# Decays counted from a chunk's first token, receptance and state split into fp16 parts, increments added before the decay

## The reference

```python
for t in range(S):
    cur = einsum('bhd,bhe->bhde', u[None] * kt, vt)
    y[:, :, t] = einsum('bhd,bhde->bhe', rt, state + cur)
    state = wt[:, :, :, None] * state + einsum('bhd,bhe->bhde', kt, vt)
```

## Time and profile before

| what | us |
|---|---|
| median of 3 runs | 421.21 |
| lowest and highest | 420.39, 424.6 |
| span of the profiled execution | 418.7 |
| busy PE, DVE, POOL, ACT | 402.8, 338.7, 187.7, 162.3 |

### The profile page before, as it was taken

How to read it: one execution, slowest core, us unless ns; L and a number is a source line. 1 busy time by engine, 2 the same in 40 slices (tenths; PEclk the granted TensorE clock), 3 DMA queues, 4 the chain that set the end, 5 groups by cost and what they waited for, 6 DMA issues and landing times.

```text
span 418.7 us, 9789 instructions
## 1 busy us (share of the span) xinstructions
PE 402.8 (96%) x3913; PEld 220.6 (53%) x3913; DVE 338.7 (81%) x561; ACT 162.3 (39%) x299; POOL 187.7 (45%) x178
## 2 busy tenths in 40 slices
PE   8999999999999999999999999999999999999981
PEld 3885555555555555555555555455453444544430
DVE  7998799998998888989989998989975787662152
ACT  3586255533343244144433433351333234321141
POOL 4445988865465655445743556464450012010000
PEclk9999999999999999999999999999999999999996
DMA  8997321468043123314430331331006189869929
GB/s 250 358 398 274 123 83 43 124 237 291 21 124 123 55 71 125 97 29 124 125 112 13 122 102 36 112 122 59 0 4 261 43 347 419 257 254 415 407 106 358
DMA packets 16541, 69.35 MB, mean 166 GB/s; under 512 B 2160, under 2 KB 3184, under 8 KB 14832
## 3 DMA queue, kind: packets, MB, share of 16 engines
q1 hardware_dynamic: 16496, 68.73, 46.9%
HBM read 64.00 MB, written 4.72 MB: 164 GB/s over the span
## 4 chain that ended last, share of the span: by engine, by line
issue 36%; PE 26%; POOL 22%; DVE 7%; DMA 5%; ACT 1%; POOLq 0%; SPq 0%; DVEq 0%
POOL att L1552 5%; DMA att<-rkT_dram 4%; POOL att L1514 4%; PE hid L578 4%; POOL att L1516 4%; PE hid L580 4%; PE hid L579 4%; POOL att L1537 3%; POOL att L1570 3%; POOL w_split L1528 3%; PE hid L846 3%; PE hid L827 1%; PE sc_ps L827 1%; DVE gated L1009 1%; PE l_ps L626 1%
## 5 line engine op out<-in xcount | busy, mean ns | idle before, releaser
L1361 ACT ACTIVATE relu<-hid,three 128x512 f32<-128x512 f32 x95 | 65.1, 686 | 136.5 <-PE hid L580 136.2
L578 PE MATMUL hid<-x_split,w_split 128*128 128x512 f16 x285 | 108.3, 380 | 0.5 <-DVE gated L1009 0.4
L580 PE MATMUL hid<-x_split,w_split 128*128 128x512 f16 x285 | 108.0, 379 | 0.0
L579 PE MATMUL hid<-x_split,w_split 128*128 128x512 f16 x285 | 108.0, 379 | 0.0
L1009 DVE SCALAR_TENSOR_TENSOR gated<-relu,hid 128x512 f32<-128x512 f32 x95 | 64.3, 677 | 22.0 <-ACT relu L1361 21.3
L1030 DVE STREAM_TRANSPOSE ring<-gated 128x512 f32<-128x512 f32 x96 | 68.3, 711 | 3.3
L1543 POOL TENSOR_TENSOR att<-att 128x1024 f16<-128x1024 f32 x20 | 40.9, 2046 | 49.1 <-ACT att L1296 49.1
L1561 POOL TENSOR_TENSOR att<-att 112x512 f32<-112x512 f32 x19 | 23.2, 1222 | 55.8 <-DVE att L928 55.8
L578 PEld LDWEIGHTS hid<-x_split,w_split 128*128 128x128 f16 x285 | 27.7, 97 | 37.3 <-DVE gated L1009 6.8
L580 PEld LDWEIGHTS hid<-x_split,w_split 128*128 128x128 f16 x285 | 27.8, 98 | 33.7
L579 PEld LDWEIGHTS hid<-x_split,w_split 128*128 128x128 f16 x285 | 27.9, 98 | 24.9 <-issue 0.3
(11 more groups left out here) (276 smaller groups left out, 759.6 us busy)
## 6 DMA issues: line engine op xcount, KB each, us to landing
att<-nat_dram SPq DMA_DIRECT2D x20, 576.0 KB, 4.2
att<-rkT_dram SPq DMA_DIRECT2D x22, 448.0 KB, 5.6
att<-wT_dram SPq DMA_DIRECT2D x22, 226.2 KB, 4.8
att<-w_dram SPq DMA_DIRECT2D x3, 1536.0 KB, 9.7
out_dram<-w_split SPq DMA_DIRECT2D x11, 384.0 KB, 3.9
att<-w_dram SPq DMA_DIRECT2D x5, 768.0 KB, 10.7
stage<-w_in_dram SPq DMA_DIRECT2D x2, 1536.0 KB, 13.2
ring<-w_outT_dram SPq DMA_DIRECT2D x1, 3072.0 KB, 15.2
```

The source lines that it names most:

```text
L578: pe.matmul(hid[s % 2][:], high, x_high, start=(q == 0), stop=False)
L579: pe.matmul(hid[s % 2][:], high, x_low, start=False, stop=False)
L580: last = pe.matmul(hid[s % 2][:], low, x_high, start=False, stop=(q == KT - 1))
L1361: nc.scalar.activation(relu_tile(s), hid[s % 2][:], ACT.Relu, bias=three[:], scale=GATE / H_SCALE)\
```

## The change

The forward scan now comes first (phase 1) and starts at `R_SCALE` from `mark`; the reciprocal of its chunk totals starts the backward scan, which comes second (phase 3). So `decay_receptance(n + 1)` moves to phase 2 of POOL and `decay_keys(n + 1)` to phase 3. The receptance product has one buffer; ACT makes its fp16 high part in phase 0 (`high_receptance`), POOL its low part in phase 0 after `diag_products` (`low_receptance`, 112 x 512). ACT saves the chunk's decay in phase 2 (`save_decay`, 112 x 4). `decay_state(n - 1)` now works on a state to which the increment was already added, still in phase 3 of POOL, and after it comes `low_state(n - 2)` (112 x 384), whose high part ACT makes in phase 2 (`high_state`, 112 x 384). `attend` replaces each fp32 product by three fp16 products of the same 96 columns.

```diff
             def attend(n):
-                pe.wait_ge(decayed, n - B + 1)
+                pe.wait_ge(state_lo_done, n - B + 1)
+                pe.wait_ge(r_lo_done, n - B + 1)
...
-                    pe.matmul(both, r_dec[n % 2][0:PD, p * P:(p + 1) * P], state[b][0:PD, p, :],
-                              start=True, stop=False, skip_group_check=True)
+                    tokens = slice(p * P, (p + 1) * P)
+                    pe.matmul(both, r_hi[0:PD, tokens], state_hi[b][0:PD, p, :], start=True, stop=False,
+                              skip_group_check=True)
+                    pe.matmul(both, r_hi[0:PD, tokens], state_lo[b][0:PD, p, :], start=False, stop=False,
+                              skip_group_check=True)
+                    pe.matmul(both, r_lo[0:PD, tokens], state_hi[b][0:PD, p, :], start=False, stop=False,
+                              skip_group_check=True)
...
+            def scan_prefix(n):
+                dve.wait_ge(w_rows_in[n % B], 16 * (n // B + 1))
+                if n:
+                    dve.wait_ge(r_dec_done, n)
+                    dve.wait_ge(decay_saved, n)
+                nc.vector.tensor_tensor_scan(prefix[0:PD, :], w_rows_of(n)[0:PD, :], mark[0:PD, :], 1.0,
+                                             ALU.mult, ALU.add).then_inc(prefix_done, 1)
...
+            def scan_suffix(n):
+                dve.wait_ge(restart_done, n + 1)
+                if n:
+                    dve.wait_ge(k_dec_done, n)
+                nc.vector.tensor_tensor_scan(suffix[0:PD, ::-1], w_rows_of(n)[0:PD, ::-1], restart[0:PD, ::-1], 1.0,
+                                             ALU.mult, ALU.add).then_inc(suffix_done, 1)
...
+            def save_decay(n):
+                act.wait_ge(prefix_done, n + 1)
+                if n >= B:
+                    act.wait_ge(decayed, n - B + 1)
+                nc.scalar.activation(chunk_decay[n % B][0:PD].rearrange("p (i o) -> p i o", o=1),
+                                     pairs(prefix[0:PD, 0:TOTAL_COLS], P + 1)[:, :, P:P + 1], ACT.Copy,
+                                     scale=1.0 / R_SCALE).then_inc(decay_saved, 1)
+            def high_receptance(n):
+                act.wait_ge(r_dec_done, n + 1)
+                if n > B:
+                    act.wait_ge(y_ready, n)
+                nc.scalar.activation(r_hi[0:PD], r_dec[0:PD], ACT.Copy).then_inc(r_hi_done, 1)
+            def high_state(n):
+                act.wait_ge(decayed, n + 1)
+                if n >= B:
+                    act.wait_ge(y_ready, n + 1)
+                nc.scalar.activation(state_hi[n % B][0:PD], state[n % B][0:PD], ACT.Copy).then_inc(state_hi_done, 1)
...
+            def low_receptance(n):
+                pool.wait_ge(r_hi_done, n - B + 1)
+                nc.gpsimd.tensor_tensor(r_lo[0:PD], r_dec[0:PD], r_hi[0:PD], ALU.subtract).then_inc(r_lo_done, 1)
...
+            def low_state(n):
+                pool.wait_ge(state_hi_done, n + 1)
+                nc.gpsimd.tensor_tensor(state_lo[n % B][0:PD], state[n % B][0:PD], state_hi[n % B][0:PD], ALU.subtract)\
+                    .then_inc(state_lo_done, 1)
...
             for n in range(B):
-                decay_keys(n + 1)
+                decay_receptance(n + 1)
...
-            decay_state(B)
-            decay_keys(B + 1)
+                if n >= 2:
+                    decay_state(n - 2)
+            low_state(0)
+            decay_state(2)
+            low_receptance(B)
+            low_state(1)
+            decay_receptance(B + 1)
             diag_products(B)
             low_scores(B)
-            decay_receptance(B + 1)
+            decay_keys(B + 1)
             diag_values(B)
...
                 if phase == 0 and is_unit(n):
                     diag_products(n)
+                    low_receptance(n)
...
                 if phase == 2:
                     if n + 1 < UNITS:
-                        decay_keys(n + 1)
+                        decay_receptance(n + 1)
                 if phase == 3:
                     if n + 1 < UNITS and n > B:
-                        decay_receptance(n + 1)
+                        decay_keys(n + 1)
                     if is_unit(n) and n > B:
                         diag_values(n)
-                    if n + 1 < UNITS:
-                        decay_state(n + 1)
+                    if n - 1 < LAST_INC:
+                        decay_state(n - 1)
+                    if n - 2 < LAST_INC:
+                        low_state(n - 2)
```

More of the change, by code:

```diff
@@ L71, in build_program @@
         suffix, prefix, restart, mark = (carve(SCAN) for _ in range(4))
-        r_dec = [carve(PB * P) for _ in range(2)]
+        r_dec = carve(PB * P)
+        r_hi, r_lo = (carve(PB * P // 2).bitcast(F16) for _ in range(2))
         k_dec = [carve(PB * P) for _ in range(2)]
@@ L116, in build_program @@
         last_max = stats[:, 7:8]
+        chunk_decay = [stats[:, i:i + PB] for i in (32, 36, 64, 68)]
+        state_hi, state_lo = ([pairs(spare[:, first + b * PB * D:first + (b + 1) * PB * D].bitcast(F16), 2 * D) for b in range(B)]
+                              for first in (2 * PB, 2 * PB + B * PB * D))
         w_early = {2: gated[:, 0:SCAN], 3: relu[:, 0:SCAN]}
@@ L251, in build_program @@
         r_dec_done = sem("r_dec_done")
+        decay_saved = sem("decay_saved")
+        r_hi_done = sem("r_hi_done")
+        r_lo_done = sem("r_lo_done")
         decayed = sem("decayed")
+        state_hi_done = sem("state_hi_done")
+        state_lo_done = sem("state_lo_done")
         state_added = sem("state_added")
@@ L479, in score @@
                         rows = slice(ALIGN * j, ALIGN * j + D)
-                        last = pe.matmul(sc_bank[j][:, cols], k_dec[n % 2][rows, cols], r_dec[n % 2][rows, cols],
+                        last = pe.matmul(sc_bank[j][:, cols], k_dec[n % 2][rows, cols], r_dec[rows, cols],
                                          start=True, stop=True)
@@ L904, in receptance_of @@
         def receptance_of(n):
-            return pairs(r_dec[n % 2][0:PD, :], P), pairs(rk_rows_of(n)[0:PD, 0:PB * P], P), \
+            return pairs(r_dec[0:PD, :], P), pairs(rk_rows_of(n)[0:PD, 0:PB * P], P), \
                 pairs(prefix[0:PD, 0:TOTAL_COLS], P + 1)[:, :, 0:P]
@@ L1124, in _ @@
             dve.wait_ge(dve_consts, 2)
[L1125 to L1126 removed]
+            nc.vector.memset(pairs(mark[:, 0:TOTAL_COLS], P + 1)[:, :, 0:1], R_SCALE).then_inc(dve_consts, 1)
             dve.wait_ge(dve_consts, 3)
             dve.wait_ge(pool_consts, 2)
+            scan_prefix(0)
+            restart_suffix(0)
             scan_suffix(0)
[L1130 to L1131 removed]
             decay_keys(0)
@@ L1411, in _ @@
             make_fold()
+            save_decay(0)
             copy_keys(0)
@@ L1415, in _ @@
             for n in range(B):
+                save_decay(n + 1)
                 if 1 <= n and n + 1 < B:
@@ L1430, in _ @@
                 if n == 2:
+                    high_state(0)
                     high_w(2)
                     scale_w(2)
+            save_decay(B + 1)
+            high_receptance(B)
+            high_state(1)
             high_v(B)
             high_scores(B)
+            high_state(2)
             for s in range(END):
@@ L1453, in _ @@
                         copy_keys(n)
+                    if n + 1 < UNITS:
+                        save_decay(n + 1)
+                    if n - 2 < LAST_INC:
+                        high_state(n - 2)
                 if s < STEPS - 1:
```

72 lines of the change are left out of this document (31 added, 41 removed).

## The result

| | before | after |
|---|---|---|
| median, us | 420.8 (4 runs beside those of after) | 437.48 (437.04 to 440.11) |
| span of the profiled execution | 418.7 | 436.1 |

The ratio is 1.040, 95% interval 1.036 to 1.044. I had forecast 427.7 and a range of 413 to 432: the direction was right, the size outside the range. Each time is about 1.7 us above the span of the same execution.

A forecast was written before the change was run, and what follows sets the result against it. It took PE and an equally long DVE, POOL, ACT loop to bind together: 2.8 + 3.9 + 3.9 - 2.9 - 1.2 = +6.5 us on 418.7, plus 2.5 from span to median, gave 427.7 us; range 413 to 432.

The forecast's parts named there:

- Two loops of one length: Per unit, PE's work and a DVE, POOL, ACT loop without PE bind together; most of PE's 11.6 us saving is lost.
- Pace of PE: In attention, three fp16 products take 0.13 us, saving 0.145 us a pair, 11.6 us for 20 units of 4 pairs.
- Conversions on POOL: The added `low_state` and `low_receptance` on POOL take 0.83 and 1.05 us, 1.88 us a unit.
- Rival 1: In plain units `low_state` takes over 0.93 us, so DVE's scan comes first and loses nothing: 422.4 us, chance 0.24.
- Seven plain units, +3.9: Seven units after the first group each get 0.55 us longer as DVE's scan meets `low_receptance`: 3.9 us.
- Gates on PE, -2.9: Four gates in units with group work, where DVE waited for PE, no longer wait: -2.9 us.
- Start of the loop, +2.8: Before the first attention product, `low_receptance(4)` and `low_state(1)` come first on POOL: 2.8 us, bounds 0 and 3.5.
- First group, +1.3 a unit: In three units with two `low_w`, POOL's idle time cannot hold all its new work: 1.3 us each, 3.9 us.
- third resource: The SBUF port: a two-input DVE instruction stands still until the running POOL product ends; a scan took 2.18 instead of 1.19 us.
- Rival 4: The port costs all it can at the start, in the first group and in plain units: +10.4, 431.6 us, chance 0.10.
- Tail, -1.2: In the last two attention units PE alone binds again, so its saving shows: -1.2 us.
- From span to median, +2.5: The median stands 2.5 us above the profiled execution's span, turning 425.2 into 427.7 us.

The follow-up runs named there:

- kernel with 128 rows: The changed kernel with the receptance's low part made over all 128 rows instead of 112, same columns: 430.13 us, ratio 1.022.
- best form: The changed kernel with the receptance's low part over 128 rows and, from unit 8 on, POOL waiting for the first scan before it: 425.52 us, ratio 1.011.
- micro kernel: A kernel of its own without the case's computation: four POOL products back to back and one DVE scan, 1.21 us alone, held to the chain's end.
- one-edit kernel: The kernel before with each fp32 product of receptance and state replaced by three fp16 products on other data: 417.57 us, ratio 0.993.
- last micro kernel: A kernel of its own: chains of POOL conversions with rows and lengths varied, and one DVE scan; it began 1.03 to 6.30 us after the tabled chains' start.

## Why the prediction was wrong, step by step

- **Two loops of one length; most of PE's saving lost: right.** 2.8 us of 11.6 arrive in the kernel before, about nothing in the kernel after.
- **Pace of PE: right** (three products in 0.13 us, 0.15 saved a pair). The Trainium skill (TensorE: Matmul & The Clock Gate, "Back-to-back issue gap") gives about 81 ns for each product of 128 columns in a stream with weight loads; for three that is 0.24 us, an estimate. The trace does not agree: its products of 96 columns, with a weight load each, start 0.04 to 0.05 apart.
- **Conversions on POOL: right**, 0.86 and 1.09 us against 0.83 and 1.05. Rival 1 (over 0.93 us) did not come about.
- **Seven plain units, +3.9: right.** 13.65 instead of 13.08, the scan 2.02 instead of 1.21; in sum +3.6.
- **Gates on PE, -2.9: nearly.** The units with group work are 2.0 us shorter in sum, 1.03 and 0.88 of it at the two largest waits.
- **Start of the loop, +2.8, and the first unit, +1.3: together 4.1, measured 6.2** (1.2 + 5.1). The first attention product starts at 46.75 (42.54 before), not at 45. `low_receptance` waited 3.65 us for ACT until 38.31, and DVE's scan in the port stretched `low_state` to 1.79 us; I had counted both POOL products bare. Removing the hold left this unit at 22.5 us (22.67 in the kernel after, 17.59 before), so it is not of the fault's making. A part of it is PE's clock, which my sum does not have. PE idles 3.5 us before this product, and in the kernel after its granted clock is 0.50 (1.2 GHz) from 46 to 52 us, where the kernel before has 1.00 throughout. The kernel with 128 rows and the best form have the same edits up to here and the same wait; from 46 to 48 us (length, busy as above, clock, DMA):

```profile
46.00:48.00 2.00, 1.11 (x21) 1.14 (x22) 1.56 (x1) 0.00 (x0) 2.00 (x2) 0.50 0.01 4
46.00:48.00 2.00, 1.37 (x40) 1.33 (x44) 1.30 (x1) 0.00 (x0) 2.00 (x2) 0.91 0.01 4
```

  The first needs 22.5 us for the unit, the second, whose clock fell later and for less long, 21.0. So 1.5 us hung on when the clock fell; that is read from one profile of each.
- **First group, +1.3 a unit: this is the step that failed.** Units 6 and 7 cost +4.5 each, 9.0 where I had 2.6. The amount of POOL work was right: with the head start removed these units cost 14.3 and 15.1 us against 13.86 before, and in the best form 15.1 twice, +1.26 each. The failed assumption is in the part on the third resource, the port: that DVE gets its turn when the running POOL product ends. I took that from one meeting, behind which POOL was idle for 1.90 us, so that nothing could run ahead. In its place the runs show a scan held through the whole line: 7.17 us each time, 7.47 in the micro kernel. Rival 4 shared the assumption, so no case of mine reached 437.
- **Tail, -1.2: wrong sign**, +0.4. I did not follow that up.
- **From span to median, +2.5: too much.** I subtracted the profiled execution's span from the median of all runs. Every run of these kernels is 1.7 to 1.8 us above its own span. The 0.8 us too much hid a little of the miss.

Sum of what was missed: 2.2 at the start, 6.4 in two units, 1.0 at the gates, 1.6 in the tail, less 0.3 in the plain units: the 10.9 us between +6.5 and +17.4 in the spans, to rounding. Undoing the head start alone brings the kernel to 430.1, inside my range.

## What to carry to other kernels

Before adding a POOL product, look at what stands behind it in POOL's queue and at its rows: one with fewer rows ahead of a line of full ones can shut DVE out of the port for the whole line. Full rows, or one wait for completion, gave back 7 us here. And where two loops have the same length, price a saving in one of them by taking that saving alone: the one-edit kernel gave 2.8 us where the busy time promised 11.6.

## What the runs showed of the hardware

- POOL's rows do not advance together; that fits all 13 chains of the last micro kernel. A product of 112 rows leaves the part for rows 112 to 127 free; it goes on to the next products and stays ahead by the whole length of the first (2.08 us for 1024 columns). 120 rows ahead of 128 gave no head start (2.21 us). What else the parts' borders are was not resolved: 96 and 64 rows ahead of 112 made the scan 0.05 us later at equal lengths. The Trainium skill (GPSIMD Engine Reference, "2.1 Instruction dispatch") says that eight cores take each instruction from a queue, each for its own 16 partitions; this agrees with 112 being a border and 120 not.
- A scan or value split of DVE, with both inputs in SBUF, enters only at a moment when no part of POOL works, by the same chains. The Trainium skill (SBUF — State Buffer, "Who interferes with whom") says that the one that issues first has the shared ports for the whole instruction. The traces agree for a single product, but show that the wait can outlast it by many: 7.17 us through four products. In the other direction POOL's next product waits for DVE each time (2.58 us instead of 1.64).
- Which instructions are held is then a matter of hundredths of a microsecond. Where ACT's scores came so late that POOL's line had a pause of 0.07 us, one scan took 2.27 us instead of 7.17; with a pause of 0.04 us (ACT's order changed, first unit) a scan took 3.70 us. Those are two units, of one profile each.
